# Mixing the later batches of an FFT mixer in couples of pairs, by three real products

## The reference, cut to what matters

```python
X = np.fft.rfft(x, axis=1)                       # x: 4 batches x 3008 x 256
Yr = Xr @ w_r - Xi @ w_i + b_r                   # w_r, w_i: 256 x 256
Yi = Xr @ w_i + Xi @ w_r + b_i
Yr = np.sign(Yr) * np.maximum(np.abs(Yr) - 0.01, 0.0)    # Yi likewise
y = np.fft.irfft(Yr + 1j * Yi, n=3008, axis=1)
h = y.reshape(12032, 256) @ w_in                 # w_in: 256 x 2048
g = np.maximum(h, 0.0) + alpha * np.minimum(h, 0.0)
return g @ w_out                                 # w_out: 2048 x 256
```

## Time and profile before

| | us |
|---|---|
| median of 3 runs | 1439.67 (1438.82 to 1443.06) |
| the profiled execution | 1440.72 |
| its span in the profile | 1438.9 |
| PE busy | 1409.9 (98%), 7230 matmuls |
| DVE busy | 908.0 (63%) |
| ACT busy | 737.8 (51%) |
| POOL busy | 275.3 (19%) |

### The profile page before, as it was taken

How to read it: one execution, slowest core, us unless ns; L and a number is a source line. 1 busy time by engine, 2 the same in 40 slices (tenths; PEclk the granted TensorE clock), 3 DMA queues, 4 the chain that set the end, 5 groups by cost and what they waited for, 6 DMA issues and landing times.

```text
span 1438.9 us, 22029 instructions
## 1 busy us (share of the span) xinstructions
PE 1409.9 (98%) x7230; PEld 1193.8 (83%) x7230; DVE 908.0 (63%) x1789; ACT 737.8 (51%) x1680; POOL 275.3 (19%) x274
## 2 busy tenths in 40 slices
PE   7999999999999999999999999999999999999997
PEld 4987888888888888888888888888888888888886
DVE  5786776666755557666765656676675555555554
ACT  3775555555544545556554445555554444444433
POOL 0432421221201421212200242112220010001000
PEclk9998999999999999999999999999999999999999
DMA  6653432221110441212211142222210111101100
GB/s 218 197 159 124 128 73 68 54 75 54 46 43 7 134 117 46 67 57 67 61 29 40 49 119 74 59 64 59 54 46 22 29 32 26 19 13 32 20 16 14
DMA packets 162861, 93.94 MB, mean 65 GB/s; under 512 B 111012, under 2 KB 140372, under 8 KB 162748
## 3 DMA queue, kind: packets, MB, share of 16 engines
q1 hardware_dynamic: 157882, 87.93, 23.0%
q10 hardware_dynamic: 4866, 4.60, 1.1%
HBM read 54.95 MB, written 37.49 MB: 64 GB/s over the span
## 4 chain that ended last, share of the span: by engine, by line
PE 93%; DVE 3%; ACT 1%; issue 1%; DMA 1%; ACTq 0%; SPq 0%; DVEq 0%
PE out_ps L413 38%; PE h_ps L413 36%; PE work_ps L413 14%; PE work_ps L506 2%; PE work_ps L447 1%; PE work_ps L507 1%; DVE turned L910 1%; ACT negpart L677 1%; PE work_ps L448 1%; DVE g_raw L863 1%; DMA x_raw<-in_x_dram 0%; PE h_ps L552 0%; DVE shrunk L834 0%; ACT above L645 0%; DVE g_lo L794 0%
## 5 line engine op out<-in xcount | busy, mean ns | idle before, releaser
L863 DVE SCALAR_TENSOR_TENSOR g_raw<-negpart,keep,h_ps 128x502 f32<-128x502 f32 (+1 forms) x384 | 282.8, 737 | 447.9 <-ACT negpart L677 442.1
L677 ACT ACTIVATE negpart<-h_ps 128x502 f32<-128x502 f32 (+1 forms) x384 | 225.7, 588 | 447.5 <-PE h_ps L413 447.1
L413 PE MATMUL out_ps<-g_hi,wout_hi 128*128 128x502 f32 (+1 forms) x768 | 309.7, 403 | 2.7 <-DVE g_lo L794 1.3
L413 PE MATMUL h_ps<-y_hi,win_hi 128*128 128x502 f32 (+1 forms) x768 | 300.5, 391 | 0.5 <-DVE y_lo L794 0.2
L413 PE MATMUL h_ps<-y_lo,win_hi 128*128 128x502 f32 (+1 forms) x768 | 300.3, 391 | 0.0
L413 PE MATMUL h_ps<-y_hi,win_lo 128*128 128x502 f32 (+1 forms) x768 | 299.6, 390 | 0.0
L413 PE MATMUL out_ps<-g_hi,wout_lo 128*128 128x502 f32 (+1 forms) x768 | 299.3, 390 | 0.0
L413 PE MATMUL out_ps<-g_lo,wout_hi 128*128 128x502 f32 (+1 forms) x768 | 298.8, 389 | 0.0
L794 DVE TENSOR_TENSOR g_lo<-g_raw,g_hi 128x502 fp32r<-128x502 f32 (+1 forms) x384 | 270.8, 705 | 0.1
L686 ACT ACTIVATE g_hi<-g_raw 128x502 fp32r<-128x502 f32 (+1 forms) x384 | 236.1, 615 | 0.3 <-DVE g_raw L863 0.3
L413 PEld LDWEIGHTS h_ps<-y_hi,win_hi 128*128 128x128 f32 x768 | 145.4, 189 | 31.9 <-DVE y_lo L794 0.8
(11 more groups left out here) (98 smaller groups left out, 1939.3 us busy)
## 6 DMA issues: line engine op xcount, KB each, us to landing
table<-in_twiddles_dram SPq DMA_DIRECT2D x32, 384.0 KB, 3.5
pair_raw<-fwd_scratch SPq DMA_DIRECT2D x96, 128.0 KB, 2.1
inv_scratch<-inv_sb SPq DMA_DIRECT2D x96, 128.0 KB, 1.7
back_raw<-inv_scratch SPq DMA_DIRECT2D x61, 192.0 KB, 2.6
x_raw<-in_x_dram SPq DMA_DIRECT2D x64, 160.0 KB
fwd_scratch<-staging SPq DMA_DIRECT2D x43, 192.0 KB, 2.1
out_dram<-turned SPq DMA_DIRECT2D x124, 40.0 KB, 2.0
out_dram<-turned SPq DMA_DIRECT2D x64, 48.0 KB, 1.9
```

The lines of the kernel that those rows point to most:

```text
L413: mm = pe.matmul(ps, lhs, rhs, start=(first and n == 0), stop=(last and n == len(terms) - 1), **kw)
L677: act.activation(negpart[:, q % 2, 0:size], h_ps[:, q % 2, 0:size], ACT.Relu, scale=-1.0).then_inc(negpart_done, 1)
L863: dve.scalar_tensor_tensor(g_raw[:, q % 2, 0:size], negpart[:, q % 2, 0:size], keep[:, m:m + 1], h_ps[:, q % 2, 0:size], ALU.mult, ALU.add ...
```

## The change

The 72 later pairs are mixed two at a time (a *couple*, p even and p odd, done when the odd one comes: `p_couple`). With s = Xr + Xi, three products serve both: s @ w_r, Xr @ (w_i - w_r), Xi @ (w_i + w_r). The real part is the first minus the third, the imaginary part the first plus the second. The weights' difference and sum are made once, by POOL, from w_r and w_i that are fetched again. A product now takes 64 columns of the even pair and 64 of the odd, so it is again 128x256 matmuls: 3 products x 2 halves x 3 = 18 for a couple.

The spectrum of a pair is now added up whole first (ACT `copy_more`, DVE `whole_spec`), then split (ACT `split_whole`, DVE `rest_whole`); the sum s is made and split by POOL, ACT and POOL again (`sum_spec`, `split_sum`, `rest_sum`). `negate`, and the negated hi copy, are gone for these pairs. Bias, threshold and splitting run once per couple on 512 columns, but the bias takes one addition of 128x512 and four of 64x256. Two `inverse2` follow one another and one copy and one store serve both. To make room, the store ring has 2 places in place of 3 (4 in place of 5 in the head), the tables of twiddles and the buffer of `load_back` are single where they were double, and one forward unit (s = 20) moves from the head into the steps.

```diff
-S_LATE = 5
+S_LATE = 4
...
-OUT_RING, OUT_HEAD = 3, 5
+OUT_RING, OUT_HEAD = 2, 4
...
+def p_couple(f, m, after):
+    p = p_unit(f, m, after)
+    return p if p is not None and p % 2 else None
...
+room = sb("room", [P, 7 * P])
+dft_raw, idft_raw = room[0:NA, 0:ROWS], room[0:ROWS, ROWS:ROWS + NA]
+spec = room[:, 0:2 * P].rearrange("p (h w c) -> p h w c", h=DH, w=2)
+spec_sum = room[:, 2 * P:3 * P].rearrange("p (h c) -> p h c", h=DH)
+bias_both = room[:, 3 * P:7 * P].rearrange("p (c e) -> p c e", c=2)
...
+mixw_hi, mixw_lo = (sb(f"mixw_{h}", [P, 3, DH, DIM], F32R) for h in ("hi", "lo"))
...
 def mix_bank(p):
...
+imag_ps, real_ps, sum_ps = work_ps[:, 1, 0:DIM], work_ps[:, 1, DIM:2 * DIM], work_ps[:, 2, 0:DIM]
...
-    return work_ps[:, p % 2, 0:DIM] if p < PAIRS else work_ps[:, 2, 0:DIM]
+    return work_ps[:, p % 2, 0:DIM] if p < PAIRS else work_ps[:, 2, p % 2 * DIM:(p % 2 + 1) * DIM]
...
+    def store_couple(p):
+        g, j = divmod(p, PAIRS)
+        sp.wait_ge(inv_copied, p + 1)
+        sp.dma_start(inv_pairs[g, :, j - 1:j + 1, :], inv_sb[:, 0:2, :]).then_inc(couple_stored, 16)
...
-        if b < 6 or v == HEAD_V:
...
+            if f == 0 and m == STEPS - 1:
+                sp.wait_ge(win_lo_done, CHUNKS)
+                sp.wait_ge(wout_lo_done, CHUNKS)
+                sp.wait_ge(itw_lo_done, GROUPS)
+                for c in range(2):
+                    sp.dma_start(ffw_raw(1)[:, c * 2 * DIM:(c + 1) * 2 * DIM].rearrange("p (h e) -> p h e", h=DH),
+                                 (w_r, w_i)[c].rearrange("(h p) e -> p h e", h=DH)).then_inc(mixw_again, 16)
+                    sp.dma_start(bias_both[:, c, :], (b_r, b_i)[c].rearrange("(o e) -> o e", o=1).to_broadcast([P, DIM])
+                                 ).then_inc(both_loaded, 16)
             if f >= 1 and 4 <= m < 10:
                 store_out(sp, f - 1, 2 * (m - 4))
...
+    def mix_couple(p):
+        if p == PAIRS + 1:
+            pe.wait_ge(mixw_lo_done, 3)
+        pe.wait_ge(spec_lo_done, p + 1)
+        pe.wait_ge(biased_done, p - 1)
+        if p % PAIRS == 1:
+            pe.wait_ge(fwd_copied, S_HEAD * (p // PAIRS + 1))
+        else:
+            pe.wait_ge(inv_copied, p - 1)
+        for ps, part, c in ((real_ps, 0, 1), (imag_ps, 1, 2), (sum_ps, 2, 0)):
+            if part == 2:
+                pe.wait_ge(sum_lo_done, p + 1 - PAIRS)
+            terms = []
+            for h in range(DH):
+                hi, lo = (three(t)[:, h, part, :, :].rearrange("p q c -> p (q c)") for t in (spec_hi, spec_lo))
+                terms += [(hi, mixw_hi[:, c, h, :]), (hi, mixw_lo[:, c, h, :]), (lo, mixw_hi[:, c, h, :])]
+            mm = product(ps, terms)
+        mm.then_inc(mix_mm, 2)
...
+                inverse2(p - 1)
                 inverse2(p)
-            p = p_unit(f, m, 1)
-            if p is not None:
-                mixing(p)
+            p = p_couple(f, m, 1)
+            if p is not None:
+                mix_couple(p)
...
+    def copy_more(p):
+        act.wait_ge(spec_mm, p + 1)
+        act.wait_ge(spec_lo_done, p)
+        if p > PAIRS:
...
+                       ACT.Copy).then_inc(more_copied, 1)
+    def split_whole(p):
+        act.wait_ge(spec_done, p - PAIRS + 1)
+        if p % 2 == 0:
+            act.wait_ge(mix_mm, p)
+        act.activation(three(spec_hi)[:, :, 0:2, p % 2, :], spec, ACT.Copy).then_inc(spec_hi_done, 1)
+    def split_sum(p):
+        act.wait_ge(sum_done, p - PAIRS + 1)
+        act.activation(three(spec_hi)[:, :, 2, p % 2, :], spec_sum, ACT.Copy).then_inc(sum_hi_done, 1)
...
+    def above_couple(p):
+        act.wait_ge(biased_done, p + 1)
+        act.wait_ge(shrunk_done, p - 1)
...
+    def split_couple(p):
+        act.wait_ge(shrunk_done, p + 1)
...
+    def copy_couple(p):
+        act.wait_ge(inv_mm, p + 1)
...
+        act.activation(inv_sb[:, 0:2, :], work_ps[:, 2, :].rearrange("p (q d) -> p q d", q=2),
+                       ACT.Copy).then_inc(inv_copied, 2)
...
+    def whole_spec(p):
+        dve.wait_ge(more_copied, p - PAIRS + 1)
+        more = room[:, 0:2 * P].rearrange("p (h c) -> p h c", h=DH)
+        dve.tensor_tensor(more, spec_views(p)[0], more, ALU.add).then_inc(spec_done, 1)
+    def rest_whole(p):
+        dve.wait_ge(spec_hi_done, p + 1)
+        rest(three(spec_lo)[:, :, 0:2, p % 2, :], spec,
+             three(spec_hi)[:, :, 0:2, p % 2, :]).then_inc(spec_lo_done, 1)
+    def bias_couple(p):
+        dve.wait_ge(mix_mm, p + 1)
+        dve.wait_ge(shrunk_done, p - 1)
+        if p == PAIRS + 1:
...
+        dve.tensor_tensor(above[:, :, :], both, bias_both, ALU.add).then_inc(mixed_done, 1)
+        dve.wait_ge(mixed_done, (p - PAIRS + 1) // 2)
+        for q in range(2):
+            at = slice(64 * q, 64 * q + 64)
+            dve.tensor_tensor(biased[0:64, q, :], above[at, 0, :], imag_ps[at, :], ALU.subtract)
+            op = dve.tensor_tensor(biased[64:128, q, :], above[at, 1, :], real_ps[at, :], ALU.add)
+        op.then_inc(biased_done, 2)
+    def shrink_couple(p):
+        dve.wait_ge(above_done, p + 1)
+        dve.wait_ge(shr_hi_done, p - 1)
...
+                                 ALU.min).then_inc(shrunk_done, 2)
...
+    def rest_couple(p):
+        dve.wait_ge(shr_hi_done, p + 1)
+        rest(shr_lo[:, :, :], shrunk[:, :, :], shr_hi[:, :, :]).then_inc(shr_lo_done, 2)
...
+    def sum_spec(p):
+        pool.wait_ge(spec_done, p - PAIRS + 1)
+        if p > PAIRS:
+            pool.wait_ge(sum_hi_done, p - PAIRS)
+            pool.wait_ge(sum_lo_done, p - PAIRS)
+        pool.tensor_tensor(spec_sum, spec[:, :, 0, :], spec[:, :, 1, :], ALU.add).then_inc(sum_done, 1)
+    def rest_sum(p):
+        pool.wait_ge(sum_hi_done, p - PAIRS + 1)
+        rest(three(spec_lo)[:, :, 2, p % 2, :], spec_sum,
+             three(spec_hi)[:, :, 2, p % 2, :]).then_inc(sum_lo_done, 1)
...
+    def make_mixw(c):
+        w = ffw_raw(1).rearrange("p (c e) -> p c e", c=2)
+        pool.wait_ge(mixw_again, 32)
+        pool.wait_ge(shr_lo_done, PAIRS)
+        pool.wait_ge(shr_hi_done, PAIRS)
+        pool.tensor_tensor((biased, shrunk)[c - 1][:, :, :].rearrange("p h e -> p (h e)"), w[:, 1, :], w[:, 0, :],
+                           (ALU.subtract, ALU.add)[c - 1]).then_inc(mixw_made, 1)
```

199 lines of the change are left out of this document (121 added, 78 removed).

## The result

| | before | after |
|---|---|---|
| median | 1439.29 (1438.82 to 1443.06, 4 runs) | 1453.32 (1453.01 to 1453.67, 4 runs) |
| ratio | | 1.0092, 95% interval 1.0074 to 1.0109 |
| profiled execution, its span | 1440.72, 1438.9 | 1453.01, 1451.2 |

The account below looks back on a forecast made before the run. PE was taken as the bound, busy 1409.9 of a 1438.9 us span. Matmuls saved (-25.9) and a wait gone (-1.9), against added waits, summed to -14.7: 1426.0 from 1440.72, or 1425.0 as a median, range 1412 to 1436.

Parts of the forecast that it names:

- the bias of a couple: Five DVE additions, then ACT's Relu, make the next negpart about 0.5 late; 0.1 us for each of 18 couples, +1.8.
- pair 19: Position 42, mixed in m = 1: g_lo ready T+6.1, PE wants it T+4.6, T ending the tile's last output; 3 x 1.4 = +4.2.
- the pairs at positions 29 and 47: Odd pairs without inverse2 or inverse1 as cover wait about 0.24 for the spectrum's lo part: +1.4 us.
- rival D: ACT's negpart and DVE's g_raw held behind waits, PE stops in hidden or output: +20, 1460 us; chance 0.06.
- 216 matmuls of 0.120: Mixing on PE: a couple takes 18 matmuls where two pairs took 24, over 36 couples: -25.9 us.
- pair 12's wait: Mixing of an even pair: its spectrum is now needed three steps after, so the 0.62 wait goes: -1.9 us.
- pair 5 (position 11) grows: Mixing of the pair behind the transposes: its existing wait of 1.09 for the spectrum's lo part grows by 0.43: +1.3 us.
- pair 9, POOL's sum: Position 20, m = 10: rest_back on POOL delays the sum's lo part for the mixing: 3 x 1.4 = +4.2 us.
- unit s = 20 and head: Forward unit moved into the steps, +0.7 for its matmuls; the head without it, -0.5: +0.2 us.
- rival B: POOL's work on the sum holds up DVE's spectrum subtraction at 36 mixings: 7 to 11 us more, 1434; chance 0.15.
- Rival A: Clean case: the added waits are hidden or share their slack, leaving -27.1, so 1412.6 us; chance 0.20.
- Rival E: SP's in-order queue is held by the single buffers of tables and load_back, pairs arrive late: +10, 1435; chance 0.06.

Follow-up runs that it names:

- run 5: Changed kernel with only ACT's Relu of a couple moved into the next step, behind negpart and g_hi, threshold unmoved: 1426.4 us, 0.991 of the kernel before.
- run 3: Changed kernel with the four 64-partition bias additions all at partitions 0 to 63, so the output is wrong: 1444.3 us, 1.0029 of the kernel before.
- run 11: Changed kernel with the Relu one step later and the first bias addition of 128x512 made twice: 1435.1 us, 0.9958 of the kernel before.
- run 4: Kernel before the change, with only the shorter store rings and unit s = 20 moved into the steps: 1440.7 us, 1.0001 of the kernel before.

## Why the prediction was wrong

The sign was wrong, and one step made it so: *the bias of a couple*. The text had the mechanism, "ACT's next negpart is late by about 0.5", and then priced it at 0.1 for each of 18 couples, +1.8, as if two steps of lag would swallow the rest. The waits of `output` for g_lo that it stands for measure +14.7, and moving the Relu out of negpart's way gives 26.9 us. The kernel without that one placement takes 1426.4, against a forecast of 1425.0. That these are so near is in part luck: in that kernel the stops at pair 19 are 1.9 us in all where 4.2 were forecast, and those of the pairs at positions 29 and 47 and for inv_sb 5.3 where 1.4 were.

It was rival D in its place and kind (ACT's negpart behind its waits, PE stopped in `output`, ten times in a batch of 12 couples), with a chance of 0.06. D's price was a wait of 1.3 us per couple and +20 on the kernel before; measured are 1.07 and +14, which is 28 above the forecast. Why the step failed, by what the runs showed:

- The delay of negpart was 0.4 in 18 couples, as the text had it, but 1.3 to 2.0 in 15. The additions themselves took 0.68 and 4 x 0.43, as forecast. But the text let the chain start right behind the mixing, and in these 15 couples DVE first waits for y_hi and then works on y and pair: the couple shown has 1.19 of waiting and 1.0 of work ahead of its first addition. The term has nothing for that.
- Two steps of lag don't swallow the delays. They add up to 38.5 us, pair 19's among them; when run 5 took them to 0, the run became 26.9 shorter, and when run 3 took 10.8 us off the chains, 9.0. The next things in ACT's list (spectrum, copy of inv_sb) are late too, and DVE, which waits for 2 us in a period of the kernel before, hides about 0.45 of another 0.69 in the step of the bias (run 11).

The step of pair 19 has a small slip of its own: T+6.1 less T+4.6 is 1.5 and not 1.4.

Term by term, per three batches:

| term | forecast | measured |
|---|---|---|
| 216 matmuls of 0.120 | -25.9 | -25.5: the 17 distances from 237.86 to 239.87 are 0.118 each |
| pair 12's wait (0.62 shown) | -1.9 | gone: -2.7 with its 0.17 and 0.1 |
| pair 5 (position 11) grows | +1.3 | +1.4 (1.81 for 1.36 per batch) |
| odd pairs at positions 29, 47 | +1.4 | +3.4 (0.55 and 0.57 per batch) |
| pair 9, POOL's sum | +4.2 | +4.7 (1.55 per batch) |
| pair 19 | +4.2 | +5.7 (1.91), and 1.9 for all three with the Relu moved |
| output for g_lo elsewhere | +1.8 | +14.7 (4.9 per batch, 9 stops) |
| mixing for inv_sb | 0 | +4.8 (1.6 per batch) |
| output for turned | 0 | +2.8 (0.93 per batch) |
| unit s = 20 and head | +0.2 | not distinguishable from 0 (run 4) |

The rest of the added stops, 1.3 per batch, is in pieces of 0.1 to 0.5. So five of the waits were found in the right places and sized within 2 us each. That wasn't enough, since the three last waits were in places where I had assumed cover. The mixing's wait for inv_sb is of this kind:

```profile
323.77 1.01 POOL L1140 TENSOR_TENSOR itw_lo<-table,itw_hi 128x384 fp32r<-128x384 f32 x1
323.92 1.40 DVE L910 TENSOR_TENSOR g_lo<-g_raw,g_hi 128x502 fp32r<-128x502 f32 x1
...
325.25 0.41 DVE L932 TENSOR_TENSOR room<-work_ps,room 128x256 f32<-128x256 f32 x1
...
326.02 0.58 ACT L746 ACTIVATE inv_sb<-work_ps 128x512 f32<-128x512 f32 x1
...
326.74 0.36 PE L461 MATMUL work_ps<-mixw_hi,spec_hi 128*128 128x256 f32 x1 [1.01 <-ACT inv_sb L746]
```

The new product for the sum shares a PSUM bank with `inverse2`, so the mixing now waits for the copy of the couple before it; that copy stands in ACT's list behind the spectrum, and the spectrum behind a g_lo of DVE that took 1.40 beside POOL's table, where it takes 0.67 otherwise. Three of the six waits for inv_sb are this one, once in each batch, with 1.0 of idle time. My rival B knew of such a collision but looked for it at the sum: every rest of the whole spectrum beside POOL's sum took 0.42 to 0.43, so B was wrong in its place. (POOL's rest of the sum did stretch the next subtraction, pair_lo, to 0.52 to 0.69 in 18 of 72 places.) The collision that cost struck where the table's inverse part had moved, to the step just ahead of its group. Rival A, 1412.6 with 0.20, is reached by no version: the best, 1420.9, still has 4.5 us of stops per batch. Rival E was wrong: in the pairs' stretch no instruction of PE, ACT or DVE waits for a transfer, and run 4 shows the shorter store rings to cost nothing.

## What to carry to other kernels

When an engine runs a written list, look for each instruction that waits for a new or longer chain at what stands behind it, and ask when that could have started. An item that waits for another engine belongs behind the steady work of the next step, and its consumer must still come after. Where two engines feed each other in turn, price such a hold near its full length, and don't count on the lag of the consumer: here 26.9 us came back for 38.5 of delay, and 9.0 for 10.8. And take the start of the chain from the list, with all that stands ahead of it there.
